# Routing logits of seven blocks moved from TensorE to VectorE, with single q/k/v buffers and SiLU in place

## The reference

```python
# attention in chunks of 32 queries: 8 memory keys + 16 left + 32 own + 8 right
scores = scale * np.matmul(q_c, k_full.transpose(0, 1, 3, 2))
a = np.exp(scores - max); a = a / (sum + 1e-09)
out[:, :, c_start:c_end] = np.matmul(a, v_full)
# feed-forward: x is 3072 x 512, w_in 512 x 2048, w_out 2048 x 512
h = x @ w_in
x = (h * (1.0 / (1.0 + np.exp(-h)))) @ w_out
# routing to the best of 8 experts (F = 1024), then that expert alone
logits = x @ w_gate + modality_bias[modality_id]
e_idx = np.argmax(logits, axis=1)
gate_w = softmax(logits)[e_idx]
out[mask] = gate_w[mask, None] * (np.maximum(x[mask] @ w1[e], 0.0) @ w2[e])
```

## Time and profile before

| | us |
|---|---|
| median of 3 runs | 1028.82 (1027.89 to 1030.62) |
| the profiled execution | 1028.19 |
| its span in the profile | 1026.5 |
| granted TensorE clock, mean | 0.98 |
| TensorE busy | 976.3 |
| VectorE busy | 308.8 |
| ScalarE busy | 354.7 |
| GpSimd busy | 302.2 |

### The profile page before, as it was taken

How to read it: one execution, slowest core, us unless ns; L and a number is a source line. 1 busy time by engine, 2 the same in 40 slices (tenths; PEclk the granted TensorE clock), 3 DMA queues, 4 the chain that set the end, 5 groups by cost and what they waited for, 6 DMA issues and landing times.

```text
span 1026.5 us, 18128 instructions
## 1 busy us (share of the span) xinstructions
PE 976.3 (95%) x6148; PEld 843.2 (82%) x6149; DVE 308.8 (30%) x749; ACT 354.7 (35%) x728; POOL 302.2 (29%) x318
## 2 busy tenths in 40 slices
PE   4799999999999999999999999993999999999997
PEld 3688888888889888888988889972788888888875
DVE  4422323223322322332332211532532322222221
ACT  4655343343343243343343322340422322222221
POOL 4677222322322232231332333221222222222222
PEclk9799999999999999999999999997899999999999
DMA  7821021421412322151241003130521111111111
GB/s 262 313 92 54 25 77 55 55 78 39 66 46 76 63 49 78 55 55 39 87 28 50 1 33 103 57 81 19 175 75 43 41 33 45 47 42 41 41 41 43
DMA packets 31257, 69.35 MB, mean 68 GB/s; under 512 B 5343, under 2 KB 9439, under 8 KB 31168
## 3 DMA queue, kind: packets, MB, share of 16 engines
q1 hardware_dynamic: 22064, 48.29, 18.3%
q0 software_dynamic: 5904, 13.57, 4.3%
q10 hardware_dynamic: 3200, 6.34, 1.9%
HBM read 55.43 MB, written 13.02 MB: 67 GB/s over the span
## 4 chain that ended last, share of the span: by engine, by line
PE 89%; DMA 6%; issue 1%; DVE 1%; ACT 1%; POOL 1%; SPq 0%; POOLq 0%; ACTq 0%; DVEq 0%
PE bank L1257 26%; PE bank L1243 26%; PE bank L1454 13%; PE bank L1323 13%; DMA token_lists<-token,slot 3%; PE bank L1228 2%; PE bank L1204 2%; DMA q_in<-q_t 2%; PE bank L1465 2%; PE bank L1288 2%; PE bank L1214 1%; PE bank L1312 1%; PE bank L1271 1%; DVE row_sum L884 0%; ACT q_bd L633 0%
## 5 line engine op out<-in xcount | busy, mean ns | idle before, releaser
L558 POOL TENSOR_TENSOR g_lo<-g_raw,g_hi 128x384 fp32r<-128x384 f32 x128 | 131.4, 1026 | 414.5 <-ACT g_hi L767 402.9
L730 ACT ACTIVATE sig<-bank 128x384 f32<-128x384 f32 x128 | 62.8, 491 | 351.5 <-PE bank L1243 351.3
L900 DVE SCALAR_TENSOR_TENSOR g_raw<-sig,bank 128x384 f32<-128x384 f32 x128 | 70.9, 554 | 365.2 <-ACT sig L730 360.0
L1243 PE MATMUL bank<-x_hi,w_hi 128*128 128x384 f32 x512 | 177.7, 347 | 0.0
L1243 PE MATMUL bank<-x_lo,w_hi 128*128 128x384 f32 x512 | 172.2, 336 | 1.0 <-issue 1.0
L1243 PE MATMUL bank<-x_hi,w_lo 128*128 128x384 f32 x512 | 173.2, 338 | 0.0
L1257 PE MATMUL bank<-w_hi,g_hi 128*128 128x512 f32 x384 | 156.7, 408 | 1.3 <-POOL g_lo L558 1.3
L1257 PE MATMUL bank<-w_hi,g_lo 128*128 128x512 f32 x384 | 151.2, 394 | 0.0
L1257 PE MATMUL bank<-w_lo,g_hi 128*128 128x512 f32 x384 | 150.9, 393 | 0.0
L1243 PEld LDWEIGHTS bank<-x_hi,w_hi 128*128 128x128 f32 x512 | 96.6, 189 | 5.2
L1243 PEld LDWEIGHTS bank<-x_lo,w_hi 128*128 128x128 f32 x512 | 96.7, 189 | 3.2
(11 more groups left out here) (165 smaller groups left out, 1251.4 us busy)
## 6 DMA issues: line engine op xcount, KB each, us to landing
k_in<-k_ctx SPq DMA_DIRECT2D x32, 384.0 KB, 4.4
v_in<-v_ctx SPq DMA_DIRECT2D x32, 384.0 KB, 3.2
w_raw<-w SPq DMA_DIRECT2D x8, 1024.0 KB, 5.5
token_rows<-y_sb ACTq DMA_DIRECT2D x8, 774.0 KB
q_in<-q_t SPq DMA_DIRECT2D x32, 192.0 KB, 3.4
w_raw<-w_in SPq DMA_DIRECT2D x4, 1024.0 KB, 7.1
w_raw<-w_out SPq DMA_DIRECT2D x4, 1024.0 KB, 8.7
list_id<-token_lists POOLq DMA_DIRECT2D x28, 0.5 KB, 2.3
```

What stands on the lines that cost most here:

```text
L558: eng.tensor_tensor(g_lo[:, f % 2, :], g_raw[:, f % 2, :], g_hi[:, f % 2, :].bitcast(F32), ALU.subtract).then_inc(g_split, 1)
L730: eng.activation(sig[:, f % 2, :], h_bank[f % 2][:, 0:BLOCK], ACT.Tanh, scale=0.5)\
L900: eng.scalar_tensor_tensor(out=g, in0=s, scalar=1.0, in1=h_bank[f % 2][:, 0:BLOCK], op0=ALU.add, op1=ALU.mult).then_inc(g_done, 1)
L1243: mm = eng.matmul(h_bank[f % 2][:, 0:BLOCK], a, b, start=(k == 0 and n == 0), stop=(k == KC - 1 and n == 2))
```

## The change

- `score(it, n)` on VectorE, for iterations 2 to 8: one instruction for each tile and expert multiplies a 128x512 tile of `y_sb` with one gate column, `wg_rows`, replicated over the partitions, and adds up the 512 products into `scored`. There are 24 in an iteration, three in each of the steps f = 3 to 10, ahead of `silu` in the step. The transposes, copies and gate matmuls of these iterations are gone from TensorE and ScalarE; iteration 9 keeps them.
- `wg_rows` (128 x 8 x 512) is filled by a DMA that replicates the transposed gate matrix, 16 KB to each of 128 partitions, on the SyncE queue behind the last four weight pieces.
- q, k and v have one buffer each instead of two. `load_ahead` orders the loads anew, and each waits until the pair before has been used. In the start stage the odd pairs use the space of `wg_rows` as their second buffer.
- Tanh writes into `g_raw` and `silu` works in place; Tanh now waits for `g_split` of two steps earlier.
- `x_raw` is gone: `rest_of_x` moves from GpSimd to VectorE and reads `o_bank` itself, behind `silu`; `values` now waits for `x_split` rather than `x_hi_done`.
- `zero_row` and `pad_ids` lie in other tiles, with the waits that this needs.

```diff
+            def load_ahead(blk, p):
+
+                nxt = (blk, p + 1) if p + 1 < PAIRS else (blk + 1, 0)
+                load_q(*nxt)
+                load_k(*nxt)
+                load_v(blk, p)
 
             eng.dma_start(wg[:, :, :], w_gate.rearrange("(k p) e -> p k e", p=P)).then_inc(consts_loaded, 16)
-            load_v(1, 0)
-            load_pairs((1, 1),)
+            load_ahead(1, 0)
             for c in range(PAIRS, 2 * CHUNKS_W):
                 load_first(c)
+            eng.wait_ge(pv_done, PAIRS)
+            eng.dma_start(wg_rows[:, :, :], w_gate_t.partition_broadcast(P)).then_inc(rows_known, 16)
             with eng.Fori(1, BLOCKS - 1) as blk:
-                load_pairs((blk, 2), (blk, 3), (blk + 1, 0), (blk + 1, 1))
-            load_pairs((BLOCKS - 1, 2), (BLOCKS - 1, 3))
+                for p in range(1, PAIRS):
+                    load_ahead(blk, p)
+                load_ahead(blk + 1, 0)
...
                 eng.wait_ge(pv_done, u + 1)
-                need(eng, x_split, u)
-                eng.activation(x_raw[:, :], o_bank[:, 0:BLOCK], ACT.Copy)
                 need(eng, l1_done, (it - 1) * FC)
                 eng.activation(x_hi[:, par, p, :], o_bank[:, 0:BLOCK], ACT.Copy).then_inc(x_hi_done, 1)
...
                         eng.wait_ge(l1_done, i + 1)
-                        need(eng, g_done, i - 1)
...
-                        eng.activation(sig[:, f % 2, :], h_bank[f % 2][:, 0:BLOCK], ACT.Tanh, scale=0.5)\
+                        need(eng, g_split, i - 1)
+                        eng.activation(g_raw[:, f % 2, :], h_bank[f % 2][:, 0:BLOCK], ACT.Tanh, scale=0.5)\
                            .then_inc(e_done, 1)
...
+            def rest_of_x(it, p, par):
+
+                eng.wait_ge(x_hi_done, it * PAIRS + p + 1)
+                eng.tensor_tensor(x_lo[:, par, p, :], o_bank[:, 0:BLOCK], x_hi[:, par, p, :].bitcast(F32), ALU.subtract)\
+                   .then_inc(x_split, 1)
...
+            def score(it, n):
+
+                t, e = divmod(n, EXPERTS)
+                if e == 0:
+                    eng.wait_ge(y_moved, (it - 2) * TT + (t + 1))
+                if isinstance(it, int) and it == 2 and n == 0:
+                    eng.wait_ge(rows_known, 16)
+                if not isinstance(it, int) or it > 2 or n > 0:
+                    eng.wait_ge(score_step, (it - 2) * TT * EXPERTS + n)
+                ins = eng.tensor_tensor_reduce(products[:, :], y_sb[:, t, 0:D], wg_rows[:, e, :], 1.0, 0.0, ALU.mult, ALU.add,
+                                               scored[:, t, e:e + 1])
+                ins.then_inc(score_step, 1)
+                if n == TT * EXPERTS - 1:
+                    eng.wait_ge(score_step, (it - 1) * TT * EXPERTS)
+                    eng.nop().then_inc(logits_done, 1)
...
+                    if route and ffn and 3 <= f < 3 + EXPERTS:
+                        for n in range((f - 3) * TT, (f - 2) * TT):
+                            score(it, n)
```

More of the change, by code:

```diff
@@ L138, in program @@
         y_sb = early("y_sb", [P, TT, ROW])
-        y_t = early("y_t", [P, TT, KC, P])
+        wg_rows = early("wg_rows", [P, EXPERTS, D])
+        scored = early("scored", [P, TT, EXPERTS])
+        products = early("products", [P, D])
         row_max = early("row_max", [P, 6])
@@ L175, in program @@
         y_out = keep("y_out", [P, 2, D])
+        y_t = keep("y_t", [P, TT, KC, P])
         cnt_i = keep("cnt_i", [1, EXPERTS], I32)
@@ L246, in steps, with last_tiles @@
             step(BLOCKS + 1, 1, False, False, True, False)
-        def tiles_at(it, f, first):
-            if isinstance(it, int) and it == BLOCKS + 1:
-                return range(TT) if f == first else ()
-            return [t for t in range(TT) if f == first + 3 * t]
+        def last_tiles(it, f, at):
+            return range(TT) if isinstance(it, int) and it == BLOCKS + 1 and f == at else ()
         def yt_bank(it, t):
-            return (pt_bank, *h_bank)[t] if isinstance(it, int) and it == BLOCKS + 1 else pt_bank
+            return (pt_bank, *h_bank)[t]
         def first_pieces(f):
@@ L646, in move_pt @@
                 need(eng, pv_done, u)
+                if isinstance(u, int) and u == 0:
+                    eng.wait_ge(zero_stored, 16)
                 for t in range(2):
@@ L744, in step @@
                             move_y(it, t)
-                    for t in tiles_at(it, f, 4) if route else ():
+                    for t in last_tiles(it, f, 4):
                         move_yt(it, t)
@@ L912, in each_tile @@
                     return row.unsqueeze(2).to_broadcast([P, TT, EXPERTS])
-                eng.wait_ge(logits_done, (it - 2) * TT + TT)
                 at = (it - 2) * TT
                 mine = bias_all[:, at:at + TT, :] if isinstance(at, int) else bias_all[:, bass.ds(at, TT), :]
-                then(eng.tensor_tensor(logit[:, :, :], o_bank[:, LOGIT:LOGIT + TT * EXPERTS]
-                                       .rearrange("p (t e) -> p t e", t=TT), mine, ALU.add))
+                if isinstance(it, int) and it == BLOCKS + 1:
+                    eng.wait_ge(last_logits_done, TT)
+                    raw = o_bank[:, LOGIT:LOGIT + TT * EXPERTS].rearrange("p (t e) -> p t e", t=TT)
+                else:
+                    eng.wait_ge(logits_done, it - 1)
+                    raw = scored[:, :, :]
+                then(eng.tensor_tensor(logit[:, :, :], raw, mine, ALU.add))
                 then(eng.tensor_reduce(lmax[:, :], logit[:, :, :], AX, ALU.max))
@@ L1017, in step @@
                         silu(i, f)
+                    if attn and 1 <= p <= PAIRS and third == 0:
+                        rest_of_x(it, p - 1, par)
                     if isinstance(it, int):
@@ L1260, in transpose_y @@
             def transpose_y(it, t):
-                n = (it - 2) * TT + t
-                eng.wait_ge(y_moved, n + 1)
-                need(eng, pt_ready, (it * PAIRS + (t + 1) if attn_now(it) else BLOCKS * PAIRS) * 2)
-                last = isinstance(it, int) and it == BLOCKS + 1
-                need(eng, yt_moved, (it - 2) * TT if last else n)
-                if last:
-                    eng.wait_ge(g_done, BLOCKS * FC)
+                eng.wait_ge(y_moved, (it - 2) * TT + t + 1)
+                eng.wait_ge(pt_ready, BLOCKS * PAIRS * 2)
+                eng.wait_ge(g_done, BLOCKS * FC)
                 for k in range(KC):
@@ L1350, in step @@
                         first_product(it, f, par)
[L1351 removed]
+                    for t in last_tiles(it, f, 5):
                         logits(it, t)
```

118 lines of the change are left out of this document (54 added, 64 removed).

## The result

| | kernel before | changed kernel |
|---|---|---|
| median, us | 1028.92 (1027.89 to 1030.62, 4 runs) | 1041.74 (1040.56 to 1043.31, 4 runs) |
| ratio | | 1.0124, 95% interval 1.0104 to 1.0144 |
| the profiled execution, us | 1028.19 | 1041.09 |
| its span, us | 1026.5 | 1039.4 |
| granted TensorE clock, mean | 0.98 | 0.963 |

What follows compares the result with a forecast made beforehand. TensorE's own list of work, and whatever starves it, was taken as the bound. From the profiled 1028.2 us, -26.5 + 5.0 + 2.1 gave 1008.8, forecast as a median of 1009 us, range 1001 to 1021.

Steps and rivals of the forecast that it cites:

- Term 1: TensorE, iterations 2 to 8: 21 tiles without transposes and gate matmuls save 1.26 us each, -26.5 us.
- Term 2: Products on VectorE: 687 ns each, 0.80 us with read and wait; VectorE keeps up, so cost 0.
- The sum for VectorE: VectorE's load in three steps: 12.0 us of 14.98, or 15.0 if each g_lo holds up a product.
- Rivals B: GpSimd's g_lo waits for a whole run of three products, 2.4 us: 1016 or 1030 us; chance 0.14.
- C: Products take two passes, 1.33 us each, and VectorE becomes the bound: 1044 us; chance 0.09.
- both readings of it: VectorE in three steps: 15.0 us with the exclusion rule in full, 12.0 without; either way no cost.
- the two meetings: VectorE and GpSimd: a COPY took 1.01 us, ending with g_lo; a g_lo begun inside a softmax product took 1.22.
- Term 3: Head of iteration 1: replicated load delays q, +5.0 us, and TensorE's lower clock after idling adds +2.1 us.
- the other loads cancel: Head of iteration 1: 576 KB more, 1.5 us, offset by the opening wait for scores coming some 1.3 us earlier.
- Rival A: Head of iteration 1: the replicated load is in nobody's way, 1002 us; chance 0.10.
- The shorter buffers cost nothing elsewhere: Single-buffer loads of pairs: released about three steps, 15 us, before use; even 11.77 us would fit, cost nothing.
- Rival D: Something behind TensorE, ScalarE's queue or the weight loads into the array, is as long: 1028 us; chance 0.03.

Runs made afterwards that it cites:

- experiment 3: Changed kernel with the load of the replicated gate columns moved behind all loads of iteration 1: 1024.24 us, ratio 1.0003.
- experiment 6: Kernel before with 59 never executed memsets in an untaken branch ahead of the last part of VectorE's program: 1033.41 us, ratio 1.0090.

## Why the prediction was wrong, point by point

**What bounds the kernel: right.** TensorE's own list, and what starves it. Everything in the middle of the pipeline is told by these two.

**Term 1, right, its window to the hundredth.** 14.98 us for three steps with routing, 20.1 us for five iterations where 18.9 were forecast (1.05 of the difference is the wait in the kernel before), and 995.98 us once the three losses are gone.

**Term 2, right, also in the price of a product.** All products of the changed kernel, in ns (least, median, greatest):

```profile
L921 DVE CUSTOM_DVE_ANT_0 products<-y_sb,wg_rows x168: 677/692/1528, 134.0 to 651.2; 128x512 f32<-128x512 f32 x168
```

The median of 692 ns stands against the 687 that were taken. The mean is 854 and the longest 1528, about twice the median: the meetings with GpSimd. In the timelines 38 of the 168 products begin while a `g_lo` runs; each of these takes 1.3 us or more, and none of the others over 0.75. The sum for VectorE had allowed for 15.0 us at most; it is busy for 12.59 of 14.98. `g_lo` takes 1029 ns in the mean, and over 1.45 us in three cases, each begun inside a product. TensorE waits for `silu` nowhere and for `g_lo` only at the head of iteration 1 (6.7 us) and once for 1.1 us, at 617.7, as in the kernel before. Rivals B (unfair meetings) and C (two passes) are out by these rows. So the rule on the exclusive port (the Trainium skill, SBUF — State Buffer, section "SBUF: two separate sides") is borne out by the lengthened products, and it cost TensorE nothing, as both readings of it had it. Of the two meetings that the prediction names beside it, only the softmax product has two inputs; the COPY has one, and the sentence on two inputs does not speak of it.

**Term 3, right in mechanism, mis-sized by a fifth.** Forecast 7.1 us, 8.4 by the trace. The chain is the one named, with the gap near 56 to 61 us, q behind the replicated load, and half clock behind it. The clock was priced rightly (2.1 us forecast; 1.9 in the nine matmuls and 0.4 in the `scores` behind them). What was off is "the other loads cancel". q landed 6.6 us later than before, at 58.79 rather than 57.5, and without the replicated load (experiment 3) it still lands 2.0 us later. From the first weights to the landing of q 2.8 MB more are moved (7.9 against 5.2), which is the replicated load and the 576 KB; but the weights start only 0.47 us earlier (37.28 against 37.75) and not 1.3. The issue of v of pair 0, which goes out ahead of them, lasts until 37.24, and the chain leads from it back to `values` (L1265, until 36.86), not to `scores`:

```profile
35.97 1.27 SPq L362 DMA_DIRECT2D v_in<-v_ctx  x1
```

Rival A is out.

**The step that failed** is the last of the sum's terms: "The shorter buffers cost nothing elsewhere: each load of a pair is released about three steps, 15 us, before its use". The release is wrong in one place. Pairs follow three steps apart from f = 2 on, but `scores` of pair 0 stand at f = 0, and from there to f = 2 it is two steps, 9.4 us, of which 8.6 are left when the buffer comes free; the description of the kernel had it ("at f = 2, 5, 8 and f = 0"). And the prediction asked whether 11.77 us, the slowest load it knew, fit into 15. In just those two steps a load takes 9.7 to 12.3 us, because of the lists' scatter, and that does not fit into 8.6. The term was put at nothing; it cost 22.0 us in the profiled run, of which 15.9 are waiting and the rest is TensorE at a low clock behind the waits.

**What the prediction had no term for** is the end: +10.2 us, shown by experiment 6 to have nothing to do with what the change computes. No rival had it either. The chance of 0.09 for slower rested on C, which did not happen: its 1044 us is the number nearest to the measured 1041.74 by accident, since no product takes two passes and TensorE does not wait for VectorE.

**Rival D** (the freed time isn't had) gave 1028 and described the outcome best in its words, but its mechanism, something that hides behind TensorE, is not what was found: in the steps themselves all the time is had.

## What to carry to other kernels

Halving a buffer moves its load into the stretch between last read and next use: look for the shortest such stretch in the whole schedule, at its seams, and for what else the DMA engines do just then, since a scatter of single words can make a 3 us load one of 12. When a change takes work off the critical engine, account for the span piece by piece with a marker in each iteration: three independent losses of 8, 22 and 10 us had hidden a gain of 26.5 here. And look at the end of the program by itself; where nothing is busy there, read the branches, before the time is put down to the change.

## What the runs showed of the hardware

**Code that is never executed changed the time.** 59 instructions in a branch not taken cost the kernel before 9 us, and 16 gave the changed kernel back about as much. In the tails a branch of VectorE takes at most 0.5 us or, when packets on an instruction queue (q14) come right behind its start, 2.1 to 4.1 us. A packet of that queue has 8 KB, 128 instructions of 64 bytes; there is a second instruction queue (q8) with packets of 16 KB (49 with 0.80 MB on the changed kernel's page), and which engines the two serve the profile does not say. In all five placements the 360 instructions of the tail loop fit one rule: counted in units of 128, the short tails have the loop in three units and the long ones in four, if the chip's numbering starts some 60 to 64 instructions ahead of the compiled program. The steady loop before it (342 instructions in the compiled program) fits the same rule: started at 1130, 1370 or 1386 no branch of VectorE's takes over 0.3 us in the trace between 840 and 900 us, started at 1189 or 1567 the jump back to the head of the loop takes about 3 us, once in a round of some 50 us. That offset is a fit, and the rule is one that no run here contradicts; more placements were not tried.

The Trainium skill, Runtime: NRT & Kernel Launch, section "Instruction fetch mechanics", says that a taken branch out of a window of two pages forces a fetch of the target before execution goes on. The branches of 2 to 4 us with their packets agree with that, though the packets behind them have 8 KB and not the 16 KB of the blocks given there. By an estimate from the sizes given there, two lines of 16 KB, a loop of 360 instructions would be short or long by units of 256; the start at 1535 is against it. With the starts at 1476 short and at 1716 long (16 less, modulo 256), 1535 would have to be short, and its tail took 13.5 us.

**The clock behind a wait.** After four of the five waits for k (2.7 to 4.2 us) TensorE's granted clock fell for some us (0.69 over 5.55 us behind the wait that ended at 288.45; 12 matmuls in 3.64 instead of 2.30 us; means of 0.83, 0.83 and 0.69 over the 10 us behind the waits that ended at 370.50, 452.75 and 535.33). Behind the one of 1.5 us, which ended at 207.11, it stayed at 1.00. Against two k buffers the five iterations lose 23.3 us for 15.9 us of waiting: the other 7.4 us are the same matmuls at the lower clock, close to half as much again as the waits.
